# A three-stage attention and expert kernel: the gate products kept in fp32 in four row groups, without split and spread, and ten weight places

## What is computed

```python
logits = x @ phi                                  # 4352 x 32
slot_input = softmax(logits, axis=0).T @ x        # 32 x 512
h = relu(slot_input[e] @ w1[e]); slot_out[e] = h @ w2[e]
x2 = softmax(logits, axis=1) @ slot_out           # 4352 x 512
e_idx = argmax(x2 @ w_gate)
h = relu(x2[mask_e] @ v1[e]); ye = h @ v2[e]      # moe2_w1, moe2_w2: 8 x 512 x 1024, 8 x 1024 x 512
out[mask_e] = gate_w * sigmoid(x2 @ w_output_gate)[e] * ye
```

## Time and profile before

| | |
|---|---|
| median of 3 runs | 509.6 us (508.0 to 510.34) |
| the profiled execution | 508.22 us, its span 506.4 us |
| PE busy in the span | 456.5 us (90%) |
| share of the span in the chain that ended last: PE | 72%, L918 alone 49% |
| the same: waiting for loads | 10% |
| ACT, DVE, POOL busy | 28%, 27%, 28% |
| granted TensorE clock, mean | 0.957 |
| moved by DMA | 88.89 MB |

### The profile page before, as it was taken

How to read it: one execution, slowest core, us unless ns; L and a number is a source line. 1 busy time by engine, 2 the same in 40 slices (tenths; PEclk the granted TensorE clock), 3 DMA queues, 4 the chain that set the end, 5 groups by cost and what they waited for, 6 DMA issues and landing times.

```text
span 506.4 us, 10287 instructions
## 1 busy us (share of the span) xinstructions
PE 456.5 (90%) x3624; PEld 256.5 (51%) x3625; DVE 137.8 (27%) x279; ACT 143.5 (28%) x330; POOL 139.5 (28%) x207
## 2 busy tenths in 40 slices
PE   6888886799978948799999999999999999999991
PEld 5676755553416625645454545545454554545440
DVE  2699898720001893201010101001010100101000
ACT  3878654301001535312121212212121221212110
POOL 3333513074000113312323323232332323233110
PEclk9999899989786978999999999999999999999997
DMA  8899446659999889777772011010101101010110
GB/s 281 279 375 306 185 168 230 272 187 413 430 426 432 343 332 393 264 253 220 250 251 94 27 45 45 27 47 25 48 28 44 45 27 44 27 48 21 42 44 2
DMA packets 29539, 88.89 MB, mean 176 GB/s; under 512 B 6174, under 2 KB 15394, under 8 KB 26432
## 3 DMA queue, kind: packets, MB, share of 16 engines
q1 hardware_dynamic: 25552, 78.06, 41.3%
q0 software_dynamic: 3952, 10.33, 6.0%
HBM read 78.14 MB, written 10.59 MB: 175 GB/s over the span
## 4 chain that ended last, share of the span: by engine, by line
PE 72%; DMA 10%; DVE 7%; issue 3%; SPq 2%; ACT 2%; POOL 2%; POOLq 0%; DVEq 0%; ACTq 0%
PE bank L918 49%; DMA arena<-in_moe_w 7%; PE bank L907 3%; PE bank L906 3%; DMA arena<-in_x 3%; PE bank L773 3%; SPq L292 2%; PE bank L821 2%; PE bank L561 1%; PE bank L550 1%; PE bank L809 1%; PE bank L574 1%; PE bank L591 1%; DVE rmx L1133 1%; DVE rsum L1164 1%
## 5 line engine op out<-in xcount | busy, mean ns | idle before, releaser
L918 PE MATMUL bank<-arena,z 128*128 x560 | 249.2, 598 | 0.9 <-DVE z L1428 0.8
L918 PEld LDWEIGHTS bank<-arena,z 128*128 128x128 f32 x560 | 103.6, 190 | 122.1 <-issue 120.0
L1428 DVE TENSOR_SCALAR z<-bank 128x512 f32<-128x512 f32 x35 | 24.2, 692 | 250.9 <-PE bank L907 250.9
L1095 ACT ACTIVATE z<-bank,tile_gate 128x512 f32<-128x512 f32 x35 | 24.0, 687 | 227.8 <-PE bank L918 227.8
L480 POOL COPY rows_to<-sidx 128x1 int32 (+1 forms) x35 | 6.4, 181 | 152.5 <-ACT z L1095 152.5
L488 POOL DMA_INDIRECT z<-token_rows,rows_from x36 | 37.9, 1054 | 29.0 <-POOL rows_from L480 29.0
L498 POOL DMA_INDIRECT out<-z,rows_to x35 | 35.7, 1019 | 29.8 <-POOL rows_to L480 29.8
L906 PE MATMUL bank<-cT,parts 128*128 128x128 bf16 x280 | 36.4, 219 | 0.5 <-issue 0.5
L907 PE MATMUL bank<-cT,parts 128*128 128x128 bf16 x280 | 36.5, 219 | 0.1
L906 PEld LDWEIGHTS bank<-cT,parts 128*128 x280 | 27.4, 98 | 1.3 <-issue 0.9
L907 PEld LDWEIGHTS bank<-cT,parts 128*128 x280 | 27.4, 98 | 1.0 <-issue 0.5
(11 more groups left out here) (228 smaller groups left out, 506.9 us busy)
## 6 DMA issues: line engine op xcount, KB each, us to landing
arena<-in_moe_w SPq DMA_DIRECT2D x31, 2048.0 KB, 12.3
arena<-in_x SPq DMA_DIRECT2D x7, 1024.0 KB, 8.5
parts<-in_moe_w SPq DMA_DIRECT2D x1, 2048.0 KB, 8.9
token_rows<-z SPq DMA_DIRECT2D x8, 162.0 KB, 2.8
arena<-in_x SPq DMA_DIRECT2D x2, 512.0 KB, 5.4
z<-token_rows,rows_from POOLq DMA_INDIRECT x36, 2.6
out<-z,rows_to POOLq DMA_INDIRECT x35
z<-in_state SPq DMA_DIRECT2D x1, 512.0 KB, 3.6
```

The lines of the kernel that those rows point to most:

```text
L918: mm = e.matmul(pY[p][:, :], hT[p][:, c, :], arena[:, bass.ds(ex * UNIT + 512 * c, 512)], start=(c == 0), stop=(c == CF - 1))
L1095: e.activation(ysb[p], pY[p][:, :], ACT.Copy, scale=tile_gate[:, q:q + 1])\
L1428: e.tensor_scalar(hT[p][:, 4:8, :], bank[2 * p + 1][:, :].rearrange("p (c t) -> p c t", c=4), 0.0, None, ALU.max).then_inc(relu_v, 1)
```

## The change

- **Gate products.** G[ex] stays as it comes out of PSUM, fp32, quarters of the columns in four row groups: ACT copies 128 x 256 once per expert to `gAll` (`keep_g`). The split, the spread, `pick`, and their semaphores are gone. G(ex) may use four PSUM banks in turn instead of two. `sort_rows` now stands behind G(7).
- **Tile loop.** The table row holds the 32 fp32 combine weights and the gate (33 words). `turn_c` is four fp32 products of 32 columns, which leave the transposed weights four times, once per row group. `hidden` is eight fp32 products over 32 rows each, in four row groups, with fixed addresses; DVE copies the expert's 128 x 256 block to one of two `gNow` buffers ahead of it (`weights_now`), with the expert from a register. `hidden` uses banks 0 to 3 for every tile and so waits for the relu of the tile before; each relu is two instructions of 256 columns instead of one of 512.
- **Weights.** `parts` gives two places, 8 and 9; place 9 is later `gAll` and `gNow`. `cT4` moves to `z2`. `SLOT` is new.
- **Table.** Three DMAs issued by ACT, between `keep_g(1)` and `keep_g(2)`, replace the 16 in SP's queue. POOL's five copies and subtractions for the split table become one copy.

The core of the diff:

```diff
-SLOT = [0, 1, 2, 5, 6, 4, 7, 3] + [8, 0, 1, 2, 5, 6, 4, 7] + [3, 5, 6, 4, 7, 3, 5, 6]
+SLOT = [0, 1, 2, 5, 6, 4, 7, 3] + [8, 9, 0, 1, 2, 5, 6, 4] + [7, 3, 8, 0, 1, 2, 5, 6]
...
             e.wait_ge(u_psum, 2)
-            for u in range(8, 21):
-                load_w(u)
-
-            e.wait_ge(row_ready, 2)
-            for b in range(NB):
-                e.dma_start(table[b * (S + NS):b * (S + NS) + S, :].rearrange("(p j) w -> p j w", j=J),
-                            rowbuf[:, J * b:J * b + J, :]).then_inc(table_out, 16)
...
-            for u in range(21, NU):
+            for u in range(8, NU):
                 load_w(u)
...
-            hidden_weights(0)
-            hidden_weights(1)
-            count_experts()
-            e.wait_ge(pick_ready, 4)
             e.wait_ge(l2_copied, 2)
-            spread(0)
-            for ex in range(2, NE):
-                if ex == NE - 2:
-                    sort_rows()
+            for ex in range(NE):
                 hidden_weights(ex)
-                spread(ex - 1)
-            spread(NE - 1)
+                if ex == 1:
+                    count_experts()
+            sort_rows()
...
             def turn_c(t, q, wait=True):
...
-                e.transpose(pC[:, 0:P], row_bf[q][:, 0:P], identb[:, :])
-                e.transpose(pC[:, P:2 * P], row_bf[q][:, NS:NS + P], identb[:, :]).then_inc(c_psum, 1)
+                for g in range(4):
+                    mm = e.matmul(pC[NS * g:NS * g + NS, :], row[q][:, 0:NS], ident[:, :], start=True, stop=True)
+                mm.then_inc(c_psum, 1)
 
             def hidden(t, p, wait=True):
-                ex = expert(t)
                 e.wait_ge(c_copied, t + 1)
+                e.wait_ge(g_copied, t + 1)
                 if wait:
-                    e.wait_ge(relu_a, t - 1)
-                    e.wait_ge(relu_v, t - 1)
-                for c in range(CF):
-                    dst = bank[2 * p + c // 4][:, P * (c % 4):P * (c % 4) + P]
-                    e.matmul(dst, gA[:, bass.ds(ex * F + P * c, P)], cT[p][:, 0:P], start=True, stop=False)
-                    mm = e.matmul(dst, gB[:, bass.ds(ex * F + P * c, P)], cT[p][:, P:2 * P], start=False, stop=True)
+                    e.wait_ge(relu_a, 2 * t)
+                    e.wait_ge(relu_v, 2 * t)
+                for h in range(2):
+                    for g in range(4):
+                        mm = e.matmul(bank[g][:, P * h:P * h + P], gNow[p][32 * g:32 * g + 32, P * h:P * h + P],
+                                      cT[p][32 * g:32 * g + 32, :], start=True, stop=True)
                 mm.then_inc(hid_psum, 1)
...
+            def weights_now(t, p):
+
+                src = texp[0:1, t:t + 1] if isinstance(t, int) else texp[0:1, bass.ds(t, 1)]
+                ex = e.value_load(src, min_val=0, max_val=NE - 1)
+                e.tensor_copy(gNow[p], gAll[:, bass.ds(ex * GW, GW)]).then_inc(g_copied, 1)
```

More of the change, by code:

```diff
@@ L71, in slot @@
         def slot(k):
-            return arena[:, k * UNIT:(k + 1) * UNIT] if k < NE else parts[:, UNIT:2 * UNIT]
+            if k < NE:
+                return arena[:, k * UNIT:(k + 1) * UNIT]
+            return parts[:, (NE + 1 - k) * UNIT:(NE + 2 - k) * UNIT]
         x_sb = [arena[:, 6 * UNIT + 2048 * q:6 * UNIT + 2048 * (q + 1)] for q in range(4)]
@@ L83, in build @@
         A = parts[:, :].rearrange("p (t c) -> p t c", t=NB * J)
-        cT4 = parts[:, 0:9 * P].rearrange("p (q t) -> p q t", q=9)
-        gA = parts[:, 0:UNIT].bitcast(BF16)
-        gB = parts[:, UNIT:2 * UNIT].bitcast(BF16)
+        gAll = parts[:, 0:NE * GW]
+        gNow = [parts[:, NE * GW + GW * q:NE * GW + GW * (q + 1)] for q in range(2)]
         z1 = sb("z1", [P, 3136])
@@ L134, in build @@
         soT = sb("soT", [P, CD, P])
-        cT = [sb(f"cT{q}", [P, 2 * P], BF16) for q in range(2)]
-        lgT = cT[0][:, :].bitcast(F32)
+        cT = [sb(f"cT{q}", [P, P]) for q in range(2)]
+        lgT = cT[0][:, :]
         ident = sb("ident", [P, P])
@@ L177, in build @@
         pCT = [bank[4], bank[5], bank[6]]
[L178 to L179 removed]
+        pG = [bank[4], bank[5], bank[0], bank[1]]
+        pC = bank[6][:, 0:P]
         pY = bank[4:6]
[L181 removed]
         zeroed, consts = sem("zeroed"), sem("consts")
@@ L444, in _ @@
             e.wait_ge(x2_psum, 2)
[L445 to L455, removed]
+            e.tensor_copy(rowbuf[:, :, 0:NS], comb).then_inc(row_ready, 1)
             e.wait_ge(sit_psum, 1)
             e.memset(hTm, 0.0).then_inc(ht_zero, 1)
[L460 to L467, removed]
             e.wait_ge(sidx_ready, 1)
@@ L820, in hidden_weights @@
                     for q in range(4):
-                        mm = e.matmul(pG[ex % 2][32 * q:32 * q + 32, 0:256], soT[:, c, 0:NS],
-                                      w[:, c, 256 * q:256 * q + 256], start=(c == 0), stop=(c == CD - 1))
+                        mm = e.matmul(pG[ex % 4][32 * q:32 * q + 32, 0:GW], soT[:, c, 0:NS],
+                                      w[:, c, GW * q:GW * q + GW], start=(c == 0), stop=(c == CD - 1))
                 mm.then_inc(g_psum, 1)
[L825 to L850, removed]
             def count_experts():
@@ L927, in step @@
                     if not isinstance(t, int) or t + 1 < ST:
-                        hidden(t + 1, (q + 1) % 2, wait=not (first and q == 0))
+                        hidden(t + 1, (q + 1) % 2)
                 output(t, q % 2, wait=not (first and q < 2))
@@ L1087, in relu @@
                     e.wait_ge(y_psum, t - 1)
-                e.activation(hT[p][:, 0:4, :], bank[2 * p][:, :].rearrange("p (c t) -> p c t", c=4), ACT.Relu)\
-                 .then_inc(relu_a, 1)
+                for g in range(2):
+                    e.activation(hT[p][:, 2 * g:2 * g + 2, :], bank[g][:, 0:GW].rearrange("p (c t) -> p c t", c=2),
+                                 ACT.Relu).then_inc(relu_a, 1)
             def gated(t, p, q, first=False):
@@ L1427, in relu, with step @@
                     e.wait_ge(y_psum, t - 1)
-                e.tensor_scalar(hT[p][:, 4:8, :], bank[2 * p + 1][:, :].rearrange("p (c t) -> p c t", c=4), 0.0, None,
-                                ALU.max).then_inc(relu_v, 1)
+                for g in range(2, 4):
+                    e.tensor_scalar(hT[p][:, 2 * g:2 * g + 2, :], bank[g][:, 0:GW].rearrange("p (c t) -> p c t", c=2),
+                                    0.0, None, ALU.max).then_inc(relu_v, 1)
+            def step(t, q, first=False):
+                relu(t, q % 2, first and q < 2)
+                with live_tile(e, live, t + 2):
+                    if not isinstance(t, int) or t + 2 < ST:
+                        weights_now(t + 2, q % 2)
             e.wait_ge(texp_ready, 2)
             live = e.value_load(texp[0:1, ST:ST + 1], min_val=NT, max_val=ST)
-            run_tiles(e, lambda t, q, first=False: relu(t, q % 2, first and q < 2), live)
-DVE_FROM = NE - 2
+            e.wait_ge(g_kept, NE)
+            for t in range(2):
+                weights_now(t, t)
+            run_tiles(e, step, live)
 WARM = 12
```

105 lines of the change are left out of this document (27 added, 78 removed).

## The result

The changed kernel takes **521.2 us** (median of 4 runs, 518.2 to 522.6) against 509.4 us before on the same chip (4 runs, 508.0 to 510.3): ratio **1.023**, 95% interval 1.0175 to 1.0277. It is slower, by 1.8 to 2.8%. The forecast was 494 us, range 485 to 506. The profiled execution took 522.6 us, its span is 520.7 us (before: 508.2 and 506.4). The kernel before was run again beside the experiments and took 508.5 us (beside e1 to e4) and 510.2 us (beside e5 to e12), so times of different groups can be off by 1 to 2 us, and the ratios count there. One execution of `e10_clock`, 501.6 us, was a slow one and is left out of its numbers.

A forecast was written before the change was run, and what follows sets the result against it. PE bounds the kernel, after waits for weight loads before the loop; two places to earn: the loop's start and the step's non-`output` time. 508.2 - 10.5 - 5 = 492.7 us for the profiled execution, 494 against the median; range 485 to 506.

The forecast's parts named there:

- part 3: Tile loop: everything in a step besides `output` falls from 1.19 to 1.05 us, -5 us over 34 steps.
- part 2: From the last gate product to the loop: output(0) starts at 205 instead of 215.5, -10.5 us.
- Part 1: Weight stream before the loop: ten places and the table on ACT keep it unbroken; `v1[7]` lands at 184.4, 13 us earlier.
- Part 2, up to `sidx`: Behind `v1[7]`: G(7) 3.5 us, the sort 2, then small DVE steps; `sidx` ready at about 191 instead of 196.0.
- Part 2, the gathers: Start of the loop: gathers start at 192.8, 195.0, 197.3; the third lands after 4 us at 201.3, output(0) at 203.
- Part 3, `turn_c`, `hidden` and the changeovers: Each step: `turn_c` 0.23 us, `hidden` 0.50 side by side, three changes of the array's division 0.32; sum 1.05 us.
- DVE idle, so its additions cost nothing: Tile loop: DVE's added register load, copy and second relu instruction fit within its 7.46 us idle per step.
- early enough: Start of the loop: `v2[0]` and `v2[1]`, queued behind `v1[7]`, need some 12 us for both and land by 197.
- Rival 1: `hidden`: a row group's weight loads aren't hidden behind its own products, +0.43 us a step, 509 us; chance 0.08.
- Rival 2: `hidden`: row groups don't run side by side, 1.71 us or more, +1.06 a step, 535 us; chance 0.08.
- point of decision: Tile loop: the change turns slower once `turn_c`, `hidden` and changeovers together exceed 1.50 us a step.
- Rival 3: Stage before the loop: no head start from the tenth place, or late gathers; -5 instead of -10.5, 499.5 us; chance 0.12.

The follow-up runs named there:

- e1: The changed kernel with PE's register load of the tile's expert moved to the head of the step, ahead of turn_c and hidden: 504.2 us, ratio to before 0.992.
- e4: The changed kernel with the early register load and the three table DMAs issued by SP between units 20 and 21: 497.8 us, ratio to before 0.979.
- e5: e4 with SP's second v2 load held until the first four gathers have landed: 511.0 us, ratio to before 1.002.
- e12: The changed kernel with a second, unused register load of the tile's expert in front of output: 542.8 us, ratio to before 1.063.
- e10_clock: e6 with 50 instead of 16 unused products ahead of the wait for the first rows: 491.4 us, ratio to before 0.958 to 0.968.
- e7: e4 with the order of places of the kernel before, so nine places and no head start: 508.3 us, ratio to before 0.998.
- e6: e4 with DVE copying the gathered weights four times side by side, so that turn_c is one transpose: 491.6 us, ratio to before 0.965.
- e2: The kernel before with the register load moved to the head of the step: 504.1 us, ratio to before 0.992.
- e8: e6 with the second v2 load held until the first four gathers have landed: 501.6 us, ratio to before 0.984.

## Why the prediction was wrong

**The step that failed is in part 3: the register load in front of `output` was priced at nothing.** The text had it "exposed for the first time" at output(0), but for the steps it said that what else moves costs nothing, and it went through DVE's instructions, not PE's. The change's own order lists showed the load still standing between `hidden` and `output`. The question to ask was what covers it when `hidden` shrinks. Its price: 8.59 - 8.08 = 0.51 us a step, 17 us in all (e1). With it out of the way the kernel is faster than before by 0.8%, and inside the range. The profiled execution was forecast at 492.7 us and took 522.6. Of these 29.9 us, 17.3 are the load, 5 the other terms of part 3, and 7.3 the gathers of part 2, all given below.

The other terms, in the prediction's order:

- **Part 1 is right, with 0.8 us of its own missing.** Units 8 and 9 are issued together at 103.22 (SP's queue above). `w2[7]` lands at 147.55 (145.4 forecast) and `v1[7]` at 187.3 (184.4), in an execution whose first `w2` unit was issued 2.1 us later than before. The chain has no wait for a weight behind `w2[7]`. The place alone is worth 10.5 us (e7).
- **Part 2, up to `sidx`: 191.6 for 191, by two errors that cancel.** `v1[7]` was 2.9 us late, and G(7), the sort and the DVE steps took 4.3 us instead of 6.6: the clock was at 1.00 over 187 to 192, where the sum had allowed for half.
- **Part 2, the gathers: wrong by 7.3 us.** The table's DMAs were priced by their wait for the gate, and their way to DRAM beside a full weight queue was left out: they landed at 195.27. The first gather came at 196.6 for 192.8. The prediction took the third gather as the last wait, at 201.3 with a landing of 4 us. The last wait was the second, issued at 198.90 and landed after 7.36 us, at 206.3, +5.0. Then came 6.0 us up to output(0) for 3.7 allowed. They hold `turn_c(1)`, `hidden(0)`, ten unused products of `keep_clock` (L504, 2.33 us at half clock), `turn_c(2)` and `hidden(1)`; the sum had only the last two, the register load, and 2 us for the clock. The Trainium skill (Trainium Kernel Development and Optimization, Key Constraints) says that DMAs of the SP, ACT and POOL queues share the same 16 engines and interleave, and that issuing from several engines saves issue time alone. The trace agrees, with 27.42 us for the last of three small transfers. Put back in SP's queue (e4), the table delays the weights instead: from `w2[7]` to `v1[7]` it is 43.1 us there and 39.8 in the changed kernel.
- **Part 3, `turn_c`, `hidden` and the changeovers: too low by 0.15 us a step**, 5 us in all, as much as the whole gain that part 3 had promised. What isn't `output`'s 6.88 was to be 1.05 us and is 8.08 - 6.88 = 1.20 (e1). The mechanism is right, since the row groups run side by side: `turn_c` and `hidden` take 0.36 + 0.66 = 1.02 us. The other 0.18 lie between the 16 records of `output` and the next `turn_c`. The timelines put 0.09 of that on the change of division: from `output`'s first product to that of `turn_c` it is 7.06 us in e1, 6.97 in e6, which has no change there, and 6.96 in the kernel before. The rest stands in the kernel before too (6.96 - 6.88), as part of the 1.19. The Trainium skill (TensorEngine Tiling (Array Packing), Key Properties) says that a change of tiling mode drains the engine; these 0.09 us agree. In all e6, with one change fewer, saves 0.25 us a step, the shorter transposes included. And the 1.19 us taken as the old price held 0.14 of the bare load (e2).
- **"DVE idle, so its additions cost nothing": right.** In the page of e1 no product of `output` waits for anything, and `hidden` (L827) has no idle time before it in the changed kernel; e6 gives DVE one copy more and gains.
- **`v2[0]` and `v2[1]` "early enough": right.** The third `v2` load, which waits for the second to land, is issued at 198.51, and the first tile, which needs `v2[1]` (e5, e8), starts at 212.3.
- **Rival 1 is refuted.** L827's sixteen weight loads, four in each row group, take 0.54 us; with bare loads of one row group it would be 0.43 more. The Trainium skill (TensorE: Matmul & The Clock Gate, Part 3) lets a load overlap products only where its row group differs; here four loads in each row group found room in those 0.54 us, beside four product records in the same row group, some 0.107 us each (an estimate: 0.43 / 4). That leaves no room for bare loads, so the measurement goes against the rule.
- **Rival 2 had the right side by the wrong mechanism.** The row groups do run side by side. Its point of decision, 1.50 us beside the 6.88 of `output`, was passed (8.59 - 6.88 = 1.71), by the bare load.
- **Rival 3** has a core of truth. Its "gathers land as late as before" cost 7 us: they landed later than before (7.36 us against 5.6 at most), behind a table that was late too.

## What to carry to other kernels

When you shorten a piece of work on an engine, look for what it was covering on **that engine's own sequencer**: a register load for an address stands in no busy column, took 1.05 us from its start to the next weight load, and can be moved ahead by one line. A small transfer that something waits for must be priced with the traffic that it meets: beside the weights it was late itself, and in their queue it made them late by 3 us. And when half of a change loses and half gains, take it apart: with the load, the table and the transpose set right, the version with this change's places and products runs in 491.6 us, where the kernel before with the same early load takes 504.1.

## What the runs showed of the hardware that was not expected

- A register load on PE: 0.30 us of TENSOR_LOAD and 0.15 of register operations, but 1.05 us until the next LDWEIGHTS. It starts ahead of its place among the products: at 236.8 in the changed kernel, as the 16 records of `hidden` ahead of it began, and at 227.6 in e1, 0.7 us into the `output` ahead of it. A second one adds 0.67 to 0.70 us (e12).
- Eight fp32 products of 32 rows and 128 columns in four row groups need 0.66 us with the changeover, as against 0.89 for 16 bf16 products over all 128 rows.
- Three DMAs of 0.56 MB together were issued by ACT beside a stream of 2 MB units of SP. The last of them took 27.4 to 27.8 us to land, in three executions.
- A change from whole products to products of 32 columns costs 0.09 us (7.06 us in e1 against 6.97 in e6).
- A gather of 128 rows lands after 2.45 us alone, and the gather in the chain took 4.85 (e10) to 7.36 us with weight loads under way.
